# The next tile's rows turned ahead of the last second products, in two PSUM banks of their own, and the experts' bounds told ahead of the tiles' slots

## The chip, the core and the metric

The kernel runs on one core of a Trainium2 chip. A core has a matrix engine (TensorE, PE in the profile; its weight loads are PEld), a vector engine (VectorE, DVE), an activation engine (ScalarE, ACT), a general engine (GpSimd, POOL) and one that issues transfers (SyncE, SP). Each has an instruction queue of its own, and they wait for each other by semaphores. A row marked PEq, DVEq, ACTq, POOLq or SPq shows what an engine's sequencer does itself: register operations, branches, semaphore waits, the issue of transfers. SBUF is the working memory of 128 partitions; PSUM has eight banks of 512 words a partition and takes the products.

The metric is the device time of the whole program in microseconds (us); lower is better.

## The reference

Three stages in a row. A linear attention with a delta rule runs over 768 steps for 4 x 8 heads of 48; its output, 3072 tokens of 384, goes through a dense layer pair (2048 wide, SiLU); then each token is either passed on as it is or gets the output of one of 8 experts (1024 wide, ReLU), weighted by its gate. The change is in the last stage:

```python
def _moe2_ref(x, w_skip, w_gate, w1, w2):
    skip_score = x @ w_skip
    do_compute = skip_score > 0
    out = x.copy()
    ...
    xc = x[do_compute]
    logits = xc @ w_gate
    e_idx = np.argmax(logits, axis=1)
    ...
    for e in range(E):
        mask = e_idx == e
        ...
        h = np.maximum(xc[mask] @ w1[e], 0.0)
        y[mask] = gate_w[mask, None] * (h @ w2[e])
    out[do_compute] = xc + y
```

## The kernel before

Attention and the dense layers are interleaved over chunks of 128 tokens until about 660 us of the profiled execution. They write each token's row (384 values and 8 logits) to a table in memory, x_table, and the token's number to id_table, at a slot in the range of its expert. Then come the experts, in tiles of G2 = 256 tokens. How many tiles each expert has is known only at run time; here it is one each, eight tiles in all.

**The plan (VectorE, lines 1552 to 1567).** One-partition instructions compute from the slots used how many tiles each expert has. They give two rows: `ends` (from which tile to which an expert runs, line 1559), which every engine reads into registers as the bounds of its loops, and `starts` (at which slot each tile begins, lines 1561 to 1567), which only POOL reads, to load a tile's ids (`load_ids_of`, line 761). One semaphore, plan_ready, tells of both; all engines wait for it. Behind the plan VectorE makes xt_lo of tile 0 (line 1570).

**Number format.** A 32-bit operand is split in two, a high and a low part (hi, lo), and each product is made of three: hi by hi, lo by hi, hi by lo (`three` for the first products; lines 1125 to 1127 for the second). ScalarE makes the high part, and VectorE the low one as the difference. For the token rows these are xt_hi and xt_lo, for the hidden layer h_hi and h_lo, for the weights w_hi and w_lo.

**A tile on each engine** (`one`, in a loop over the tiles of an expert, within a loop over pairs of experts; the last two experts stand behind that loop):
- TensorE runs n from 0 to 9. For n < 8 it makes a group of nine first products (w1, 128 of the 1024 columns) in the bank up_ps[n % 2], for n >= 2 a group of six second products (w2) of d = n - 2 into both down_ps. Group n of the first products waits for h_lo of group n - 2, since it takes that group's bank. At n = 8 and n = 9 it first turns half of the next tile's rows (`transposes`: three transposes for each half, by a product with the identity, line 1096) into up_ps[0] and up_ps[1], which no first product needs any more, and then makes the second products of d = 6 and d = 7.
- ScalarE makes h_hi from each group (line 1254), the high parts of the next expert's weights in between (line 1137, w_hi), at n = 2 a copy of the gathered rows (xg), and at the end both xt_hi of the next tile (`xt_parts`). A tile begins with a small operation that brings a table load with it where the pair loop begins (line 1249: three of the eight tiles).
- VectorE makes h_lo (line 1584), the low parts of the next expert's weights (line 1537), the gate, then both xt_lo of the next tile, and last y of this tile in two instructions (line 1602), once all second products are done (edown_done). After that its sequencer goes through the loop's end and reads the next expert's bounds (lines 513, 514) before the next h_lo.
- POOL gathers by indirect DMA the rows of the next tile (line 739), loads the ids of the one after (line 735), and scatters y to the output (line 794). `hold` is a wait followed by a one-element operation (line 684), so that what is behind it in the queue starts late enough. Ahead of the loops it loads the ids of tiles 0 and 1 and gathers the rows of tile 0 (lines 760 to 768); the turned rows of tile 0 are made another way and don't need that gather, but ScalarE's copy in tile 0 does, and POOL gathers tile 1 only when that copy is done.
- SP loads the weights of the expert after next, piece by piece, each as VectorE has split the piece before it in the same buffer (line 650).

In each engine the order of the work is the order of the code, with waits written by hand.

## Time and profile before

| | us |
|---|---|
| median of 3 timed runs | 834.72 (834.37 to 834.73) |
| the profiled execution | 832.83 |
| its span, first to last instruction | 831.2 |
| TensorE busy | 785.8 (95%) |
| VectorE busy | 568.4 (68%) |
| ScalarE busy | 369.3 (44%) |
| POOL busy | 112.3 (14%) |

Tile 0 of the experts begins at 670.08 us, the last tile's products end at about 818.7, and the last rows of the output are stored by 831.2. In the rows further down, a time in front is the start from the beginning of the span, the second number the duration; `[0.21 <-DVE xt_lo L1576]` says that the engine sat idle for 0.21 us before and what released it. A row with x3 merges three instructions, and its duration runs from the first's start to the last's end. Neighbouring instructions of one engine overlap in the records, so a start minus the start before is the pace. L and a number is a line of the kernel before; kv_t holds y, the gates and the scattered rows in this stage, kq_t the gathered rows, bp and dg the weights as loaded, u_sb the plan's rows.

### The profile page before, as it was taken

To read this page: it belongs to the slowest core of one execution; us is meant where nothing else is said; L and a number is where in the kernel's file an instruction comes from. 1 tells how busy PE (TensorE), PEld (TensorE's weight loads), DVE (VectorE), ACT (ScalarE), POOL (GpSimd) and SP (SyncE) were. 2 spreads that over 40 slices of the span, in tenths; PEclk is the share of its full clock that TensorE was granted. 3 is DMA by queue.
4 is the path that set the end of the run, shared out by engine and by line. 5 is a ranking of instruction groups with operands and counts; after the bars stand their busy time and mean duration, and the time that the engine had idled before them with its cause. 6 is when DMAs were issued, how large, how long until landed. Compare 5 with 4: busy or idle time off the path is not lost.

```text
span 831.2 us, 29093 instructions
## 1 busy us (share of the span) xinstructions
PE 785.8 (95%) x12081; PEld 714.4 (86%) x12082; DVE 568.4 (68%) x1504; ACT 369.3 (44%) x1042; POOL 112.3 (14%) x281
## 2 busy tenths in 40 slices
PE   5977999999999999999999999999999989999993
PEld 3545888899989998899999899999999989999993
DVE  6978798868687776778768677655323666767751
ACT  3723433535335343453424444343543565666641
POOL 1000000001020000101002010100104054344441
PEclk9987999999999999999999999999999999999997
DMA  8753121122201213122220211211123646655510
GB/s 270 231 163 124 34 67 53 60 91 66 86 34 66 69 63 100 39 65 72 68 89 24 67 61 48 65 41 47 40 78 122 196 141 196 192 191 185 188 32 15
DMA packets 46649, 79.75 MB, mean 96 GB/s; under 512 B 5680, under 2 KB 35082, under 8 KB 46144
## 3 DMA queue, kind: packets, MB, share of 16 engines
q1 hardware_dynamic: 43104, 73.07, 27.3%
q0 software_dynamic: 3424, 4.93, 1.9%
q8 instruction: 92, 1.51, 0.8%
q14 instruction: 29, 0.24, 0.1%
HBM read 67.05 MB, written 13.19 MB: 97 GB/s over the span
## 4 chain that ended last, share of the span: by engine, by line
issue 79%; POOL 9%; DMA 6%; POOLq 2%; PE 2%; DVE 1%; SPq 0%; ACT 0%
DMA id_table<-token,slot 5%; POOL idle L684 3%; POOL kq_t L739 2%; POOL id_table L729 2%; PE psum L984 1%; POOL ids_all L735 1%; POOL out L794 1%; DMA x_sb<-kq 1%; DMA id_table<-x_sb 0%; POOLq L513 0%; POOLq L514 0%; POOLq L761 0%; PE psum L840 0%; POOL token L722 0%; PE psum L985 0%
## 5 line engine op out<-in xcount | busy, mean ns | idle before, releaser
L1018 PE MATMUL psum<-xt_hi,w_hi 128*128 128x256 f32 x768 | 225.9, 294 | 7.1 <-issue 2.7
L1019 PE MATMUL psum<-xt_lo,w_hi 128*128 128x256 f32 x768 | 217.2, 283 | 0.0
L1020 PE MATMUL psum<-xt_hi,w_lo 128*128 128x256 f32 x768 | 217.0, 283 | 0.0
L1194 ACT ACTIVATE h_raw<-psum 128x256 f32<-128x256 f32 x192 | 73.8, 385 | 309.2 <-PE psum L1020 307.5
L1453 DVE TENSOR_TENSOR h_lo<-h_raw,h_hi 128x256 fp32r<-128x256 f32 x192 | 81.3, 424 | 160.7 <-ACT h_hi L1195 149.8
L1018 PEld LDWEIGHTS psum<-xt_hi,w_hi 128*128 128x128 f32 x768 | 144.8, 189 | 16.8 <-issue 10.8
L1020 PEld LDWEIGHTS psum<-xt_hi,w_lo 128*128 128x128 f32 x768 | 146.0, 190 | 0.0
L1019 PEld LDWEIGHTS psum<-xt_lo,w_hi 128*128 128x128 f32 x768 | 145.4, 189 | 0.0
L1042 PE MATMUL psum<-w_hi,h_hi 128*128 128x394 f32 x384 | 138.7, 361 | 3.0 <-DVE h_lo L1453 2.4
L1044 PE MATMUL psum<-w_hi,h_lo 128*128 128x394 f32 x384 | 131.2, 342 | 0.0
L1043 PE MATMUL psum<-w_lo,h_hi 128*128 128x394 f32 x384 | 131.0, 341 | 0.0
L684 POOL TENSOR_TENSOR idle<-half 1x1 f32<-1x1 f32 x125 | 35.3, 296 | 641.6 <-PE psum L916 484.7
L1137 ACT ACTIVATE u_sb<-psum 32x96 f32<-32x96 f32 (+1 forms) x360 | 88.7, 247 | 25.5 <-PE psum L916 20.5
L1042 PEld LDWEIGHTS psum<-w_hi,h_hi 128*128 128x128 f32 x384 | 72.4, 188 | 9.9 <-DVE h_lo L1453 4.2
L1387 DVE SCALAR_TENSOR_TENSOR bp<-psum,gamma,seen 128x256 f32<-128x256 f32 x192 | 79.2, 475 | 2.4 <-PE psum L1005 2.3
L1195 ACT ACTIVATE h_hi<-psum 128x256 fp32r<-128x256 f32 x192 | 72.6, 378 | 0.0
L1043 PEld LDWEIGHTS psum<-w_lo,h_hi 128*128 128x128 f32 x384 | 72.4, 189 | 0.0
L1044 PEld LDWEIGHTS psum<-w_hi,h_lo 128*128 128x128 f32 x384 | 72.3, 188 | 0.0
L1408 DVE TENSOR_TENSOR inv<-inv,outer 128x30 f32<-128x30 f32 (+9 forms) x180 | 59.9, 333 | 6.2
L1137 ACT ACTIVATE w_hi<-bp 128x768 fp32r<-128x768 f32 (+1 forms) x62 | 58.5, 944 | 9.5 <-DMA bp<-moe_w_in 9.5
L1537 DVE TENSOR_TENSOR w_lo<-bp,w_hi 128x1024 fp32r<-128x1024 f32 (+1 forms) x48 | 52.4, 1092 | 14.8 <-ACT w_hi L1137 14.8
L1405 DVE TENSOR_TENSOR outer<-low,inv 128x30 f32<-128x30 f32 (+9 forms) x180 | 58.8, 327 | 2.9
(183 smaller groups left out, 1100.5 us busy)
## 6 DMA issues: line engine op xcount, KB each, us to landing
kq_t<-kq SPq DMA_DIRECT2D x24, 512.0 KB, 3.6
bp<-moe_w SPq DMA_DIRECT2D x24, 512.0 KB, 5.7
kv_t<-kv SPq DMA_DIRECT2D x24, 384.0 KB, 3.1
bp<-moe_w SPq DMA_DIRECT2D x24, 384.0 KB, 5.1
kd<-kq SPq DMA_DIRECT2D x20, 256.0 KB
x_table<-x_sb SPq DMA_DIRECT2D x13, 392.0 KB, 2.9
out<-x_sb SPq DMA_DIRECT2D x12, 384.0 KB
bp<-moe_w_in SPq DMA_DIRECT2D x6, 512.0 KB, 7.1
```

The lines of the kernel that those rows point to most:

```text
L684: return g.tensor_tensor(idle[:, at:at + 1], half[0:1, 0:1], half[0:1, 0:1], ALU.mult)
L1018: m(out, hi, x_hi, start=first, stop=False)
L1019: m(out, hi, x_lo, start=False, stop=False)
L1020: return m(out, lo, x_hi, start=False, stop=last)
L1042: m(down_ps[a][:, 0:WS], h_hi[:, r, rows], w_hi[1][:, w], start=i == 0, stop=False)
L1043: m(down_ps[a][:, 0:WS], h_hi[:, r, rows], w_lo[1][:, w], start=False, stop=False)
L1044: last = m(down_ps[a][:, 0:WS], h_lo[:, r, rows], w_hi[1][:, w], start=False, stop=i == M1 - 1)
L1137: return a_.activation(out, in_, ACT.Copy, scale=scale)
L1194: a_.activation(h_raw[i % 2][:, :], up_ps[i % 2][:, 0:G2], ACT.Silu)
L1195: a_.activation(h_hi[:, i % RING, :], up_ps[i % 2][:, 0:G2], ACT.Silu).then_inc(h_hi_ready, 1)
L1387: d.scalar_tensor_tensor(bp[t % NB][:, h, :], gram_ps(t, h), gamma[quad(t)][:, at:at + 1], seen[:, h // 2, :], ALU.mult, ALU.mult).then_in ...
L1453: d.tensor_tensor(h_lo[:, i % RING, :], h_raw[i % 2][:, :], f32(h_hi[:, i % RING, :]), ALU.subtract).then_inc(h_lo_ready, 1)
```

## The change

Two banks of PSUM that the expert stage didn't use (6 and 7) take the turned rows (turn_ps), in place of up_ps[0] and up_ps[1]. TensorE turns both halves at n = 8, ahead of the wait for h_lo and of the second products of d = 6; nothing stands ahead of those of d = 7 any more but their own wait. ScalarE and VectorE read the turned rows from the new banks, in the same order among their instructions as before.

In the plan, `ends` is told by plan_ready as soon as it is there, VectorE then makes xt_lo of tile 0, and only behind that come the instructions that compute `starts`, which have a semaphore of their own, starts_ready. POOL waits for that one ahead of line 761.

```diff
@@ -182,6 +182,7 @@
         psum = ctx.enter_context(nc.psum_tensor("psum", [P, 8, 512], F32))
         up_ps = [psum[:, g, :] for g in range(2)]
         down_ps = [psum[:, 2 + g, :] for g in range(2)]
+        turn_ps = [psum[:, 6 + g, 0:KD * C] for g in range(2)]
         first_ps = psum[:, 4:6, :].rearrange("p b (k n) -> p (b k) n", n=G2)
 
 
@@ -251,7 +252,7 @@
             sem, ("route_step", "route_in", "token_ready", "id_stored", "table_blank"))
         out_stored, table_stored = sem("out_stored"), sem("table_stored")
 
-        plan_step, plan_ready = sem("plan_step"), sem("plan_ready")
+        plan_step, plan_ready, starts_ready = map(sem, ("plan_step", "plan_ready", "starts_ready"))
         ids_loaded, xg_gathered, xg_copied, ids_copied = map(sem, ("ids_loaded", "xg_gathered", "xg_copied", "ids_copied"))
         ew_half, ew_split = map(sem, ("ew_half", "ew_split"))
         ew_loaded = [sem(f"ew_loaded{x}") for x in range(len(e_stage))]
@@ -761,7 +762,7 @@
                 load_ids(pool.value_load(starts[0:1, bass.ds(t, 1)], min_val=0, max_val=E * N - G2), ids_in, ids_loaded)
 
             load_ids(0, ids_next, first_in)
-            pool.wait_ge(plan_ready, 1)
+            pool.wait_ge(starts_ready, 1)
             load_ids_of(1)
             pool.wait_ge(table_stored, 16 * NP)
             pool.wait_ge(out_stored, 16 * NP)
@@ -1093,7 +1094,7 @@
             def transposes(t, a):
                 pe.wait_ge(xg_gathered, t * 32 + 32)
                 for x in range(KD):
-                    last = tr(up_ps[a][:, C * x:C * x + C], xg_in[a][:, C * x:C * x + C], ident[:, :])
+                    last = tr(turn_ps[a][:, C * x:C * x + C], xg_in[a][:, C * x:C * x + C], ident[:, :])
                 last.then_inc(xgt_ps[a], 1)
 
             def one(e, i, more):
@@ -1112,13 +1113,14 @@
                                 last = three(up_ps[n % 2][:, 0:G2], w_hi[i][:, w], w_lo[i][:, w], xt_hi[0][:, x, :], xt_lo[0][:, x, :],
                                              x == 0, x == KD - 1)
                             last.then_inc(eup_done, 1)
+                        if n == M2:
+                            for a in range(2):
+                                transposes(t + 1, a)
                         if n >= 2:
                             d = n - 2
                             pe.wait_ge(eh_lo_ready, t * M2 + d + 1)
                             if d == 0:
                                 pe.wait_ge(y_ready, t + 1)
-                            if n >= M2:
-                                transposes(t + 1, n - M2)
                             w = slice(W2_AT + DM * d, W2_AT + DM * d + DM)
                             for a in range(2):
                                 rows, r = slice(C * a, C * a + C), d % RING
@@ -1239,7 +1241,7 @@
             def xt_parts(t):
                 for a in range(2):
                     act.wait_ge(xgt_ps[a], t + 1)
-                    cp(xt_hi[0][:, :, C * a:C * a + C], up_ps[a][:, 0:KD * C].rearrange("p (k c) -> p k c", k=KD)).then_inc(xgt_hi[a], 1)
+                    cp(xt_hi[0][:, :, C * a:C * a + C], turn_ps[a].rearrange("p (k c) -> p k c", k=KD)).then_inc(xgt_hi[a], 1)
 
             def one(e, i, more):
                 first, last_t = expert_bounds(act, e)
@@ -1556,7 +1558,12 @@
             then(d.tensor_scalar(tiles_f, tiles_f, 1.0, None, ALU.max))
             then(d.tensor_tensor(part, earlier, tiles_f.unsqueeze(1).to_broadcast([1, E + 1, E]), ALU.mult))
             then(d.tensor_reduce(ends_f, part, AX.X, ALU.add))
-            d.tensor_copy(ends, ends_f)
+            d.tensor_copy(ends, ends_f).then_inc(plan_ready, 1)
+
+            for b in range(2):
+                dve.wait_ge(xgt_hi[b], 1)
+                d.tensor_tensor(xt_lo[0][:, FIRST[b]:FIRST[b + 1], :], first_ps[:, FIRST[b]:FIRST[b + 1], :],
+                                f32(xt_hi[0][:, FIRST[b]:FIRST[b + 1], :]), ALU.subtract).then_inc(xgt_lo[b], 1)
 
             then(d.tensor_scalar(jump, tiles_f[:, 0:E - 1], -float(G2), float(N), ALU.mult, ALU.add))
             then(d.tensor_tensor(past, tile_no[0:1, :].unsqueeze(2).to_broadcast([1, MAXT + 2, E - 1]),
@@ -1564,16 +1571,11 @@
             then(d.tensor_tensor(past, past, jump.unsqueeze(1).to_broadcast([1, MAXT + 2, E - 1]), ALU.mult))
             then(d.tensor_reduce(starts_f, past, AX.X, ALU.add))
             then(d.scalar_tensor_tensor(starts_f, tile_no[0:1, :], float(G2), starts_f, ALU.mult, ALU.add))
-            d.tensor_scalar(starts, starts_f, float(E * N - G2), None, ALU.min).then_inc(plan_ready, 1)
-            for b in range(2):
-                dve.wait_ge(xgt_hi[b], 1)
-                d.tensor_tensor(xt_lo[0][:, FIRST[b]:FIRST[b + 1], :], first_ps[:, FIRST[b]:FIRST[b + 1], :],
-                                f32(xt_hi[0][:, FIRST[b]:FIRST[b + 1], :]), ALU.subtract).then_inc(xgt_lo[b], 1)
-
+            d.tensor_scalar(starts, starts_f, float(E * N - G2), None, ALU.min).then_inc(starts_ready, 1)
             def xt_parts(t):
                 for a in range(2):
                     dve.wait_ge(xgt_hi[a], t + 1)
-                    d.tensor_tensor(xt_lo[0][:, :, C * a:C * a + C], up_ps[a][:, 0:KD * C].rearrange("p (k c) -> p k c", k=KD),
+                    d.tensor_tensor(xt_lo[0][:, :, C * a:C * a + C], turn_ps[a].rearrange("p (k c) -> p k c", k=KD),
                                     f32(xt_hi[0][:, :, C * a:C * a + C]), ALU.subtract).then_inc(xgt_lo[a], 1)
 
             def one(e, i, more):
```

TensorE, the end of a tile in the last expert, before: kq_t0 and kq_t1 are the two halves of the next tile's gathered rows.

```order
L1127 MATMUL psum<-w_hi1,h_lo 128x384
L1117 REGISTER_ALU
L1094 ISA
L1096 MATMUL psum<-ident,kq_t0 128x128 x3
L1125 MATMUL psum<-w_hi1,h_hi 128x384
L1126 MATMUL psum<-w_lo1,h_hi 128x384
L1127 MATMUL psum<-w_hi1,h_lo 128x384
L1125 MATMUL psum<-w_hi1,h_hi 128x384
L1126 MATMUL psum<-w_lo1,h_hi 128x384
L1127 MATMUL psum<-w_hi1,h_lo 128x384
L1117 REGISTER_ALU
L1096 MATMUL psum<-ident,kq_t1 128x128 x3
```

And the same place of the changed kernel, whose lines have moved by one to two:

```order
L1129 MATMUL psum<-w_hi1,h_lo 128x384
L1095 ISA
L1097 MATMUL psum<-ident,kq_t0 128x128 x3
L1097 MATMUL psum<-ident,kq_t1 128x128 x3
L1121 REGISTER_ALU
L1127 MATMUL psum<-w_hi1,h_hi 128x384
L1128 MATMUL psum<-w_lo1,h_hi 128x384
L1129 MATMUL psum<-w_hi1,h_lo 128x384
L1127 MATMUL psum<-w_hi1,h_hi 128x384
L1128 MATMUL psum<-w_lo1,h_hi 128x384
L1129 MATMUL psum<-w_hi1,h_lo 128x384
L1121 REGISTER_ALU
```

The second half's three transposes have moved ahead of the six second products of d = 6; the twelve second products now stand together, and no instruction has gone or come.

VectorE, the end of the plan, before: L1559 writes `ends`, L1567 `starts`, both in u_sb.

```order
L1559 CAST u_sb<-u_sb 1x9
L1561 TENSOR_SCALAR u_sb<-u_sb 1x7
L1562 TENSOR_TENSOR h_raw<-tile_no,u_sb 1x154
L1564 TENSOR_TENSOR h_raw<-h_raw,u_sb 1x154
L1565 TENSOR_REDUCE u_sb<-h_raw 1x22
L1566 SCALAR_TENSOR_TENSOR u_sb<-tile_no,u_sb 1x22
L1567 TENSOR_SCALAR u_sb<-u_sb 1x22
L1570 TENSOR_TENSOR xt_lo<-psum,xt_hi 128x512
L1570 TENSOR_TENSOR xt_lo<-psum,xt_hi 128x256
```

The same place of the changed kernel:

```order
L1561 CAST u_sb<-u_sb 1x9
L1565 TENSOR_TENSOR xt_lo<-psum,xt_hi 128x512
L1565 TENSOR_TENSOR xt_lo<-psum,xt_hi 128x256
L1568 TENSOR_SCALAR u_sb<-u_sb 1x7
L1569 TENSOR_TENSOR h_raw<-tile_no,u_sb 1x154
L1571 TENSOR_TENSOR h_raw<-h_raw,u_sb 1x154
L1572 TENSOR_REDUCE u_sb<-h_raw 1x22
L1573 SCALAR_TENSOR_TENSOR u_sb<-tile_no,u_sb 1x22
L1574 TENSOR_SCALAR u_sb<-u_sb 1x22
```

Both xt_lo, which wait for ScalarE's xt_hi, have moved ahead of the six instructions that make `starts`.

## Rows read from the trace of the kernel before

**Rows 1.** Lines, 640 us to the end, TensorE: busy, mean ns | idle before, releasers.
```profile
L1018 PE MATMUL psum<-xt_hi,w_hi 128*128 128x256 f32 x218 | 62.9, 288 | 5.3 <-issue 2.7 <-DVE xt_lo L1576 1.5 <-DVE h_lo L1584 1.0
```

**Rows 2.** Timeline, TensorE, from tile 2 to tile 3: start us, us, line, [idle before].
```profile
723.77 0.49 PE L1096 MATMUL psum<-ident,kq_t 128*128 128x128 f32 x3
...
725.15 0.49 PE L1096 MATMUL psum<-ident,kq_t 128*128 128x128 f32 x3
...
726.36 0.34 PE L1127 MATMUL psum<-w_hi,h_lo 128*128 128x384 f32 x1
...
726.91 0.36 PE L1018 MATMUL psum<-xt_hi,w_hi 128*128 128x256 f32 x1 [0.21 <-DVE xt_lo L1576]
...
729.15 0.39 PE L1018 MATMUL psum<-xt_hi,w_hi 128*128 128x256 f32 x1
```

**Rows 3.** Timeline of VectorE there; then its queue's register operations: ns, first and last start.
```profile
725.24 0.56 DVE L1576 TENSOR_TENSOR xt_lo<-psum,xt_hi 128x384 fp32r<-128x384 f32 x1
726.20 0.56 DVE L1576 TENSOR_TENSOR xt_lo<-psum,xt_hi 128x384 fp32r<-128x384 f32 x1 [0.41 <-ACT xt_hi L1137]
726.84 1.14 DVE L1602 SCALAR_TENSOR_TENSOR kv_t<-psum,kv_t,kq_t 128x384 f32<-128x384 f32 x2
728.67 0.42 DVE L1584 SCALAR_TENSOR_TENSOR h_lo<-psum,h_hi 128x256 fp32r<-128x256 f32 x1 [0.69 <-ACT h_hi L1254]
...
L1581 DVEq ALU_OP  x1: 40/40/40, 726.9 to 726.9; - x1
...
L1581 DVEq FUSED_REGOPS  x1: 63/63/63, 728.5 to 728.5; - x1
```

**Rows 4.** The same from tile 1 to tile 2, where the pair loop goes round.
```profile
707.93 1.14 DVE L1602 SCALAR_TENSOR_TENSOR kv_t<-psum,kv_t,kq_t 128x384 f32<-128x384 f32 x2
710.42 0.83 DVE L1584 SCALAR_TENSOR_TENSOR h_lo<-psum,h_hi 128x256 fp32r<-128x256 f32 x2 [1.35 <-ACT h_hi L1254]
...
L1581 DVEq FUSED_REGOPS  x1: 63/63/63, 710.0 to 710.0; - x1
```

**Rows 5.** Timeline of VectorE, then of ScalarE, at the hand-over to tile 0.
```profile
666.11 0.16 DVE L1559 CAST u_sb<-u_sb 1x9 int32<-1x9 f32 x1
666.19 0.15 DVE L1561 TENSOR_SCALAR u_sb<-u_sb 1x7 f32<-1x7 f32 x1
...
667.60 0.17 DVE L1567 TENSOR_SCALAR u_sb<-u_sb 1x22 int32<-1x22 f32 x1
667.69 1.00 DVE L1570 TENSOR_TENSOR xt_lo<-psum,xt_hi 128x512 fp32r<-128x512 f32 x2
...
666.51 0.60 ACT L1137 ACTIVATE xt_hi<-psum 128x512 fp32r<-128x512 f32 x1 [5.05 <-PE psum L1086]
667.37 0.38 ACT L1137 ACTIVATE xt_hi<-psum 128x256 fp32r<-128x256 f32 x1 [0.27 <-PE psum L1086]
```

**Rows 6.** POOL's queue at L761, then the timelines of POOL and SP.
```profile
L761 POOLq TENSOR_LOAD <-u_sb x1: 520/520/520, 668.4 to 668.4; - x1
...
670.49 0.36 POOL L684 TENSOR_TENSOR idle<-half 1x1 f32<-1x1 f32 x2
...
672.79 1.01 POOL L739 DMA_INDIRECT kq_t<-x_table,ids_all  x1 [0.30 <-issue]
...
675.93 0.67 POOL L684 TENSOR_TENSOR idle<-half 1x1 f32<-1x1 f32 x1 [2.13 <-DMA kq_t<-x_table,ids_all]
...
680.85 1.00 POOL L739 DMA_INDIRECT kq_t<-x_table,ids_all  x1 [0.31 <-issue]
...
686.56 0.33 POOL L684 TENSOR_TENSOR idle<-half 1x1 f32<-1x1 f32 x2 [3.96 <-DMA kq_t<-x_table,ids_all]
...
675.28 9.61 SPq L650 DMA_DIRECT2D bp<-moe_w  x6
```

**Rows 7.** Timeline of TensorE: the start of tile 0, and its stop near the end.
```profile
670.08 0.36 PE L1018 MATMUL psum<-xt_hi,w_hi 128*128 128x256 f32 x1 [2.75 <-issue]
...
686.54 0.55 PE L1096 MATMUL psum<-ident,kq_t 128*128 128x128 f32 x3 [1.15 <-DMA kq_t<-x_table,ids_all]
```

## The prediction

> **What bounds the kernel now.** I read the page of the profile first: TensorE is busy for 95% of the span, so only its gaps and the work it waits for can move the time. The grouped lines of the stretch after 640 us then show how little it waits in the experts: 5.3 us ahead of the first products of a group, 2.7 of them "issue", 1.5 behind xt_lo and 1.0 behind h_lo [rows 1]. Third, the timeline of TensorE over one change of tile. The first transposes start at 723.77, the second at 725.15, the last second product at 726.36, the next tile's first product at 726.91, and its third group of first products (n = 2) at 729.15 [rows 2]. That last start is the one to watch. At every one of the eight tiles the third group starts 0.06 us after the first h_lo ends; here h_lo starts at 728.67 and takes 0.42, so it ends at 729.09. Two groups lie between 726.91 and 729.15, and both run without a break, so a tile that begins earlier gains only if its first h_lo comes earlier too.
>
> Fourth, VectorE and its queue at the same place [rows 3]. The two y instructions (L1602) start at 726.84, about 0.14 after the last product's modelled end (726.36 + 0.34). The queue's first register operation at the loop's end follows at 726.9, and the last one of the next tile's head at 728.5. h_lo starts at 728.67, 0.17 later. So the chain from tile to tile is: last second product, y, 1.7 us of register work of VectorE's queue (the bounds are read again for every expert), first h_lo, third group. xt_lo, which the change brings forward, stands beside this chain and not on it.
>
> Last, the hand-over to tile 0: VectorE's plan, ScalarE's xt_hi and POOL's queue [rows 4 to 6].
>
> **The turning of the next tile, part by part.** No instruction is added: six transposes, twelve second products, two xt_hi, two xt_lo, two y. On TensorE three transposes and six products take 725.15 - 723.77 = 1.38, three transposes and five products 726.36 - 725.15 = 1.21; so a product is 0.17 and a transpose about 0.12. All six first take 0.7, and the last product, with eleven ahead of it, starts where it did, at 726.36.
>
> The second transposes end about 1.05 earlier, so the second xt_hi does too, and the second xt_lo follows the first (725.24) at once, 0.48 later, and ends near 726.28 instead of 726.76. TensorE can then go on at 726.53 instead of 726.91: 0.38 per change of tile, seven times. I count none of it directly. y waits for the last product, which hasn't moved, so VectorE's queue is ready when it was: 728.5 plus the operation and a dispatch, about 728.60. h_lo can start 0.07 earlier than 728.67, and TensorE waits the rest at the third group. At the two changes where the pair loop goes round, ScalarE loads a table and holds h_lo longer: y 707.93, last register operation 710.0, h_lo 710.42 [rows 4]; the other one reads alike, with 0.48 in place of 0.42 between the last two. ScalarE starts its table load about 0.9 earlier, since it has both xt_hi behind it, and h_lo falls back on VectorE's queue, 0.3 earlier. At the other five changes h_lo now starts 0.1 to 0.27 after the last register operation, of which about 0.13 can't go: 0 to 0.14 each, together 0.4. Sum: 2 x 0.3 + 0.4 = **1.0 us gained**. If that queue were quicker by a tenth per tile it would be 1.7, if ScalarE's table load still held h_lo, 0.4. The last tile gains nothing: its y waits for the same last product.
>
> **The bounds ahead of the slots.** plan_ready is told after L1559 (starts 666.11, 0.16 long) and not after L1567 (667.60): 1.5 us earlier. Then VectorE waits for xt_hi: ScalarE's two copies are 666.51 + 0.60 and 667.37 + 0.38, ended 667.11 and 667.75 [rows 5]. xt_lo runs from 667.13 to 668.17 (1.00 for the two before, and a little between them), 0.5 earlier than 668.69. TensorE, whose queue now reads the bounds while its last products of the hand-over run, can begin near 668.6 and not at 670.08 [rows 7]. It then meets the same wall: VectorE's queue must pass the six plan instructions left, and so is 0.2 to 0.4 earlier with the first h_lo. And all of it is lost at the end of this tile, where TensorE stands for 1.15 us until the rows of tile 1 land, 686.54 [rows 7]. Worth there: 0.
>
> **What is paid.** The six plan instructions (L1561 to L1567, 666.19 to 667.77, 1.58) now stand behind both xt_lo: they start at 668.09 and end at 669.67. POOL waits for them (starts_ready) ahead of L761, which began at 668.4 [rows 6]. It begins at 669.7: **1.3 later**. Behind it in POOL's queue are the load of tile 1's ids, the gather of tile 0's rows (second half issued at 672.79, landed 675.93), the copy by ScalarE, and the gather of tile 1's rows (second half 680.85, landed 686.56); POOL waits only for these landings on the way, so all shift by 1.3. TensorE's stop at 686.54 becomes 687.84. Behind ScalarE's waiting copy are the fourth h_hi and the weight splits of the next expert; they come 1.3 later too, and TensorE may stop for some 0.4 at the sixth group, but it has that to spare before 687.84. So its gap there is about 2.3 us, less than the 2.75 before 670.08 [rows 7], after which the first product takes 0.36 as at every change of tile [rows 2]; I expect no loss of clock.
> Ends for this cost: nothing, if the gather of tile 0 is held by something else after all; above, 1.3 plus what the weight loads add. The first gather landed 2.1 after its second half had been issued (672.79 + 1.01 long, to 675.93), with no other transfer about; the second, among the weight loads, took 4.7 (680.85 + 1.00, to 686.56). SP issues the first of these loads at 675.28 [rows 6], and the moved gather is issued until 675.1. It could take up to 2.6 more, 3.9 in all. I take 1.4, near the quiet row, as the loads start only when most of its bytes have moved.
> The Trainium skill, DMA: Bandwidth & Descriptors, section Queues, rings and completion order, says that each DMA engine takes turns between its queues packet by packet. By that, a gather that meets the loads is slowed from the first shared packet; the two gathers of rows 6 agree (2.1 and 4.7), and it speaks for the upper end.
>
> **Sum**: -1.0 + 1.4 = +0.4 us on the profiled execution (832.83, span 831.2). The median of the timed runs is 834.72, 1.9 above that execution; the step carries over, and gives 835.1.
>
> **The rivals.**
> 1. The early start counts in full (faster). If VectorE's queue could do its register work while y still waits, the first h_lo would follow h_hi. Then five changes give 0.38 each, and the two with a table load about 0.85, as h_hi behind the earlier table load then sets them; 3.6 in all, less 1.3: 832.4. Against it: at the changes of tile the register operation stands 0.06 to 0.1 after y's start, never before. A chance of 0.08.
> The Trainium skill, Advanced Engine Details and Errata, section Sequencer Loop, has engine instructions waiting in a queue while control instructions go on; by that this rival would win. In rows 3 the register operation at 726.9 does follow y at 726.84, which had a semaphore to wait for, so the row speaks against the rule here.
> 2. The gather falls among the weight loads (slower). The place is the gather of tile 0, the price up to 3.9 in place of 1.4, and it decides once the landing is late by more than 2.7: then the sum passes +1.7. For it: the loads at 675.28. Against: its second half would be written by 675.1, and the loads are paced by splits that shift as well. With 3.8 it gives 837.5. A chance of 0.16; a fallen clock behind the longer stop would add to it.
> 3. The later slots cost nothing (the gather is held by the landing of ids). Then only the 1.0 stays: 833.7. Against: POOL's two holds ahead of that gather stand back to back at 670.49, with no wait between them [rows 6]. A chance of 0.08.
> The forecast has 0.68.
>
> **How the numbers follow.** What a measurement of this kernel can tell is about 0.2%, 1.7 us: faster is below 833.05, slower above 836.39. The forecast (834.2 to 836.2 by its bounds) and nearly all of rival 3 are within; rival 1 is faster, rival 2 mostly slower. That makes 0.11 faster, 0.70 the same, 0.19 slower. The range, 833.3 to 837.2, takes in rival 3 and most of rival 2.
>
> **What would show it.** Right: six transposes together at about 0.7 us, last product and y at the same distance behind them as before; the next tile's first product directly behind the last second product; a new wait of about 0.3 to 0.4 for h_lo ahead of each tile's third group; y to first h_lo still 1.75 to 1.85, and about 2.2 with the pair loop; L761 of POOL near 669.7, TensorE's stop for the rows of tile 1 ending near 687.9. Wrong: h_lo less than 1.7 behind y, no wait at the third group, or L761 near 668.4. If that stop ends after 689.3, rival 2 has it.

## The result and the profile after

| | kernel before | changed kernel |
|---|---|---|
| median, timed side by side (20 runs each) | 833.39 us (830.19 to 835.3) | 835.0 us (833.46 to 838.52) |
| ratio, changed to before | | 1.0027, 95% interval 1.0015 to 1.0039 |
| profiled execution (its span) | 832.83 (831.2) | 835.72 (834.1) |
| TensorE busy | 785.8 | 786.3 |

By the ratio the change costs some 2.3 us. The gain at the changes of tile came out as worked; the loss at tile 0 is more than twice what I had put down.

**A change of tile.** TensorE and VectorE from tile 2 to tile 3, which answer to [rows 2, 3], and then the register operations of VectorE's queue (ns, first and last start):

```profile
727.36 0.82 PE L1097 MATMUL psum<-ident,kq_t 128*128 128x128 f32 x6
...
729.95 0.33 PE L1129 MATMUL psum<-w_hi,h_lo 128*128 128x384 f32 x1
...
732.66 0.39 PE L1019 MATMUL psum<-xt_hi,w_hi 128*128 128x256 f32 x1 [0.24 <-DVE h_lo L1586]
```

```profile
728.83 1.02 DVE L1578 TENSOR_TENSOR xt_lo<-psum,xt_hi 128x384 fp32r<-128x384 f32 x2
730.42 1.14 DVE L1604 SCALAR_TENSOR_TENSOR kv_t<-psum,kv_t,kq_t 128x384 f32<-128x384 f32 x2 [0.58 <-PE psum L1129]
732.18 0.42 DVE L1586 SCALAR_TENSOR_TENSOR h_lo<-psum,h_hi 128x256 fp32r<-128x256 f32 x1 [0.61 <-ACT h_hi L1256]
...
L1583 DVEq ALU_OP  x1: 40/40/40, 730.5 to 730.5; - x1
...
L1583 DVEq FUSED_REGOPS  x1: 63/63/63, 732.1 to 732.1; - x1
```

The two xt_lo run without a pause, y waits for the last product, the register work starts behind it and ends at 732.1, h_lo follows 1.76 behind y, and TensorE, which is ready earlier, waits 0.24 for it. From third group to third group the eight tiles were 18.92, 18.25, 18.90, 18.28, 18.25 and 18.27 apart before, behind tile 1, and are now 18.60, 18.19, 18.59, 18.16, 18.25 and 18.10.

**Tile 0**, which answers to [rows 5 to 7]. VectorE, POOL's queue and POOL, SP, TensorE:

```profile
665.92 0.16 DVE L1561 CAST u_sb<-u_sb 1x9 int32<-1x9 f32 x1
666.96 1.07 DVE L1565 TENSOR_TENSOR xt_lo<-psum,xt_hi 128x512 fp32r<-128x512 f32 x2 [0.88 <-ACT xt_hi L1139]
...
669.36 0.17 DVE L1574 TENSOR_SCALAR u_sb<-u_sb 1x22 int32<-1x22 f32 x1
...
672.18 1.22 DVE L1539 TENSOR_TENSOR w_lo<-bp,w_hi 128x1024 fp32r<-128x1024 f32 x1
```

```profile
L762 POOLq TENSOR_LOAD <-u_sb x1: 520/520/520, 669.6 to 669.6; - x1
...
672.38 1.97 POOL L740 DMA_INDIRECT kq_t<-x_table,ids_all  x1 [0.41 <-issue]
674.66 1.01 POOL L740 DMA_INDIRECT kq_t<-x_table,ids_all  x1 [0.30 <-issue]
678.65 0.18 POOL L685 TENSOR_TENSOR idle<-half 1x1 f32<-1x1 f32 x1 [2.99 <-DMA kq_t<-x_table,ids_all]
...
683.56 1.74 POOL L740 DMA_INDIRECT kq_t<-x_table,ids_all  x1 [0.30 <-issue]
...
688.98 0.33 POOL L685 TENSOR_TENSOR idle<-half 1x1 f32<-1x1 f32 x2 [2.72 <-DMA kq_t<-x_table,ids_all]
...
673.60 12.88 SPq L651 DMA_DIRECT2D bp<-moe_w  x6
```

```profile
668.41 0.36 PE L1019 MATMUL psum<-xt_hi,w_hi 128*128 128x256 f32 x1 [1.25 <-DVE xt_lo L1565]
...
671.91 0.39 PE L1019 MATMUL psum<-xt_hi,w_hi 128*128 128x256 f32 x1 [1.13 <-DVE h_lo L1586]
...
680.33 0.39 PE L1019 MATMUL psum<-xt_hi,w_hi 128*128 128x256 f32 x1 [1.78 <-DVE h_lo L1586]
...
688.96 1.03 PE L1097 MATMUL psum<-ident,kq_t 128*128 128x128 f32 x6 [1.98 <-DMA kq_t<-x_table,ids_all]
...
690.10 0.52 PE L1128 MATMUL psum<-w_lo,h_hi 128*128 128x384 f32 x1
690.42 0.52 PE L1129 MATMUL psum<-w_hi,h_lo 128*128 128x384 f32 x1
```

Read from the top: the bounds are told earlier, tile 0 starts 1.67 earlier than in [rows 7] (0.18 of it is chance: this execution came to the hand-over that much sooner), and the slots are made behind xt_lo; POOL reads them at 669.6. But SP's first weight load has come forward too, from 675.28 to 673.60, before the gather is written. The gather's first half now takes 1.97 in place of 1.07, and its rows land 2.7 later than in [rows 6]. Of the early start little is left at once: TensorE waits 1.13 for h_lo ahead of tile 0's third group, as foreseen. It then stops twice more, 1.78 for h_lo at the sixth group and 1.98 for the rows of tile 1, and behind the last stop its second products stand 0.32 apart and not 0.17. The stretches of that place show why (us, busy time of each engine, granted clock of TensorE, share of DMA, GB/s):

```profile
688.00:690.00 2.00, 1.04 (x7) 1.05 (x8) 0.31 (x3) 0.46 (x1) 0.63 (x4) 0.89 0.87 234
690.00:692.00 2.00, 2.00 (x7) 2.00 (x7) 1.04 (x2) 0.71 (x3) 0.58 (x1) 0.50 0.53 177
692.00:694.00 2.00, 2.00 (x12) 2.00 (x12) 0.36 (x1) 0.00 (x0) 0.00 (x0) 0.76 0.02 1
```

A granted clock of 0.50 is the lower of the two levels, 1.2 GHz. Before the fall TensorE had stood still for 1.98. In the profile shown of the kernel before, the same place stands at 1.00. From the six transposes to y it is 4.68 here and 3.06 at the change of tile above: 1.6 for the clock.

### The profile page after: what moved, and what is told of

It reads as the page before. It is cut to its first block, busy times and chain, and to the rows that moved or that the text cites. A ratio compares the mean times of both kernels' runs of the same rounds, so it can differ in the third digit from the quotient of the medians.

```text
span 834.1 us, 29085 instructions
## 1 busy us (share of the span) xinstructions
PE 786.3 (94%) x12081; PEld 716.4 (86%) x12082; DVE 567.7 (68%) x1504; ACT 368.5 (44%) x1042; POOL 114.3 (14%) x281
## 4 chain that ended last, share of the span: by engine, by line
PE 65%; issue 14%; DVE 8%; POOL 6%; DMA 2%; POOLq 2%; ACT 2%; SPq 0%; ACTq 0%; DVEq 0%
PE psum L1043 9%; PE psum L1019 8%; PE psum L1045 7%; PE psum L1044 7%; PE psum L1021 7%; PE psum L1020 7%; DVE bp L1389 3%; PE psum L917 3%; PE psum L875 2%; POOL idle L685 2%; POOL kq_t L740 2%; PE psum L931 2%; DMA bp<-moe_w_out_t 2%; PE psum L895 2%; PE psum L841 2%
```

## The experiments

Each was timed in five rounds beside the kernel before, except where it says otherwise. Executions differ in when the hand-over to the experts comes (660.11 to 668.05 in these profiles, with nothing of the change ahead of it), so tile 0 is compared from one product on, called the hand-over here: the first of the twelve of L1086 (up to L1089 in the other kernels), the last that TensorE makes ahead of tile 0. The columns from "first gather issued" to "third group of tile 1" are us behind it:

| kernel | hand-over at | first gather issued | its rows land | rows of tile 1 land | third group of tile 1 | clock at 0.50 in tile 0 | ratio |
|---|---|---|---|---|---|---|---|
| before | 664.48 | 6.93 | 11.45 | 22.1 | 27.50 | nowhere | 1 |
| before, again | 666.57 | 7.15 | 11.60 | 23.2 | 28.61 | at the start of tile 0 | |
| turning alone | 667.47 | 7.10 | 11.56 | 22.9 | 28.24 | at the start | 0.9982 |
| turning alone, again | 662.90 | 7.16 | 12.46 | 23.6 | 30.47 | behind the stop | 0.9983 |
| turning, gather delayed a little | 660.11 | 7.21 | 11.63 | 20.8 | 27.32 | at the start | 0.9982 |
| turning, gather delayed | 662.55 | 8.14 | 15.04 | 24.4 | 30.04 | behind a stop | 0.9995 |
| turning, y at the head | 663.20 | 7.18 | 12.48 | 23.6 | 30.11 | behind the stop | 0.9952 |
| y at the head alone | 664.32 | 7.30 | 11.70 | 23.3 | 29.08 | at the start | 1.0034 |
| **changed** | 664.30 | 8.08 | 14.35 | 24.7 | 31.57 | behind a stop | 1.0027 |
| plan alone | 665.42 | 8.16 | 14.83 | 25.1 | 30.50 | behind a stop | 1.0027 |
| changed, loads held | 664.16 | 8.14 | 13.45 | 24.8 | 31.59 | behind a stop | 1.0022 |
| changed, slots first | 668.05 | 8.03 | 15.07 | 26.0 | 31.39 | behind a stop | 1.0044 |
| slots first, loads held | 667.23 | 8.40 | 13.78 | 25.3 | 32.23 | behind a stop | 1.0046 |
| y at the head, slots first, loads held | 666.93 | 8.40 | 13.81 | 25.3 | 31.85 | behind a stop | 1.0015 |

**1. The turning alone, and the plan alone.** Each is the kernel before with one half of the diff.

> The kernel before with only the two banks and the early transposes; plan and semaphores as before. Theory A (the change of tile is held by VectorE's register work between y and the first h_lo; the loss of the whole change sits in tile 0 and comes from the plan): third group to third group shrinks by 0.3 us at the two changes with a table load and by 0 to 0.15 at the others, about 1.0 in all; tile 0 starts near 670.1 and its stop for the rows of tile 1 ends near 686.5, as before; the clock stays at 1.00. Time about 1.0 us (0.1%) below before, 'same' by the bound. Theory B (the early transposes themselves cost, for instance the clock falls because all products stand together): slower than before, with a granted clock under 1.00 in tile 0. Rival of the forecast (the early start counts in full): 3 us below.

> The kernel before with only the plan part: ends told first, xt_lo, then starts with a semaphore of its own; transposes in the old place. Theory A: all of the loss is here. The whole change's trace had the third group of tile 1 3.9 us later than before; I expect 3.5 to 4 here too, SP's first weight load near 673.6 in place of 675.3, the gather of tile 0's rows landing near 678.6, TensorE's stop ending near 689, and a granted clock of 0.5 behind it; time about 3.5 us (0.4%) above before, so about 1 above the whole change. Theory B (the loss comes with the turning): no more than 1.4 above.

Measured: turning 832.42, ratio 0.9982 (0.9966 to 0.9998), and run once more 0.9983 (0.9961 to 1.0004); plan 836.19, ratio 1.0027 (1.0009 to 1.0044). The gain is the turning's, and the plan loses 2.3 alone, less than the 3.5 expected. Beside the turning it loses 1.0027 against 0.9982, 3.7 us. The turning's tile 0 was not that of the kernel before, as I had expected: its clock fell in both profiles (table).

> The turning alone once more, on the same chip as turn_y_head. The first profile of it had a lowered clock in the first products of tile 0 (0.86 granted from 668 to 680). Expected: ratio 0.998 again, 1.0 to 1.6 below the kernel before; the periods from third group to third group 18.6 and 18.2 again, and, if the clock was chance, the tile 0 of the kernel before (27.5 from first own product to the third group of tile 1).

**2. Weight loads held until the gather has landed.**

```diff
             sp.wait_ge(plan_ready, 1)
+            sp.wait_ge(xg_gathered, 32)
```

> The whole change, and SP waits until the rows of tile 0 have landed before it issues the first weight load of the loop. Theory A (the earlier start of tile 0 brings the weight loads 1.7 us forward, into the gather that the plan has made 1.3 later): the gather of tile 0 lands about 1.3 to 1.5 later than before (677.3), POOL's gather instruction takes 1.0 and not 1.97, the gather of tile 1 lands near 688, TensorE's stops together are under 3 us and the clock stays at 1.00; about 1.5 to 2.5 us below the whole change. Theory C (the gather is late only because starts are late, the loads don't matter): the landing stays near 678.6 and the time is that of the whole change, or later because the loads are.

```profile
672.30 1.94 POOL L741 DMA_INDIRECT kq_t<-x_table,ids_all  x1 [0.47 <-issue]
674.55 1.01 POOL L741 DMA_INDIRECT kq_t<-x_table,ids_all  x1 [0.30 <-issue]
677.61 0.18 POOL L686 TENSOR_TENSOR idle<-half 1x1 f32<-1x1 f32 x1 [2.05 <-DMA kq_t<-x_table,ids_all]
```

This is POOL with the loads held (first load at 678.88). The landing behind the second half takes 2.05 and not 2.99: the loads cost the gather 0.9. But the first half is as long as in the changed kernel, and the loads now fall into the gather of tile 1, which lands when it did. Ratio 1.0022 (1.0005 to 1.004): nothing won of the 1.5 to 2.5 expected.

**3. The slots first again, with the bounds still told early**, once with the loads free and once held.

```diff
             d.tensor_copy(ends, ends_f).then_inc(plan_ready, 1)
-            for b in range(2):          # both xt_lo
-                ...
             then(d.tensor_scalar(jump, tiles_f[:, 0:E - 1], -float(G2), float(N), ALU.mult, ALU.add))
             ...
             d.tensor_scalar(starts, starts_f, float(E * N - G2), None, ALU.min).then_inc(starts_ready, 1)
+            for b in range(2):          # both xt_lo
+                ...
```

> The whole change with xt_lo of tile 0 behind starts again, ends still told first: starts ready at 667.8 as before, all engines read their bounds 1.5 us earlier. Theory A: POOL's load of starts is back at 668.4; TensorE can begin tile 0 near 668.9, so the weight loads still come forward, by about 1.2; they then meet a gather that is 1.3 earlier than in the whole change, and collide less: its landing near 676 to 677, TensorE's stop ending near 686.5 to 687.5, clock 1.00. Time 2.5 to 3.5 us below the whole change, about 0.5 to 1 below before. Theory C (only starts matter): the same with the landing at 675.9 exactly as before.

> The changed kernel with two differences: the six instructions that make the slots run ahead of xt_lo again (the bounds still told before them), and SP waits for the gathered rows of tile 0 (xg_gathered at 32) ahead of its first weight load. It is the fourth corner of a square: slots early or late, weight loads among the gather or behind it. Theory A, the early weight loads cost: the gather lands about 2.1 us behind the issue of its second half, not 5.7 as in slots_first; TensorE's stop for the rows of tile 1 ends near 22.5 to 23 behind its first own product of the hand-over (before 22.1, changed 24.7, slots_first 26.0), the clock stays up, and the time is 1.5 to 2.5 below the changed kernel: near 832.5 to 833.5, ratio about 0.9995 to the kernel before. Theory B, the loads are only moved into the gather of tile 1, which pays it back: the first gather lands quickly, the second takes 5 or more, the stop ends near 24.5 as in loads_held, and the time is near 835.5, ratio 1.002.

Measured: 837.1, ratio 1.0044 (1.002 to 1.0069), and 835.93, ratio 1.0046 (1.0023 to 1.0069). Both theories of the first failed, and theory A of the second; its theory B (1.002) was nearer. Early bounds with the slots first lose at least as much as the whole edit. But the gather is as late as before (issued at 8.03 and 8.40), so no run here has early bounds and a gather on time. POOL of the kernel with the loads held, and its transfers from 671.7 to 673.3 (queues: packets, MB, share):

```profile
671.95 0.59 POOL L737 DMA_DIRECT2D ids_all<-id_table  x1
673.29 0.56 POOL L737 DMA_DIRECT2D ids_all<-id_table  x1 [0.75 <-issue]
...
674.90 0.18 POOL L686 TENSOR_TENSOR idle<-half 1x1 f32<-1x1 f32 x1 [0.85 <-DMA ids_all<-id_table]
675.63 1.90 POOL L741 DMA_INDIRECT kq_t<-x_table,ids_all  x1 [0.55 <-issue]
...
q8 instruction: 1, 0.02, 4.0%
```

In [rows 6] the two holds ahead of the gather begin at 670.49, 1.92 behind the issue of tile 0's ids, and end without a wait for them. Here the second hold waits, until 2.95 behind that issue; with the loads free it was 3.27, with y at the head 3.12. In those 1.6 us one packet of 16 KB is read by the queue that brings instructions, while the ids come; in the kernel before no such packet stands in the same stretch, it comes 1.1 to 1.7 later. The other profiles divide the same way. In all six with early bounds that packet starts 4.9 to 5.5 behind the hand-over, and the ids land 2.9 to 3.2 behind their issue; in all eight with the old bounds it starts 6.6 to 7.3 behind it, and they land in 2.0 to 2.3. That the packet holds back the ids is likely, but only argued: no run moved it alone. In the changed kernel the ids were late too (landed 7.27 behind the hand-over), but the hold for them began at 7.49, so there they cost nothing. These three profiles came late to the hand-over (666.9 to 668.1), as did one of the turning alone (667.47); that is ahead of anything that differs.

**4. A late gather with the old bounds.** The turning alone, and idle operations of POOL ahead of the load of tile 1's ids (seven, then thirteen).

```diff
             pool.wait_ge(plan_ready, 1)
+            for _ in range(13):
+                hold(plan_ready, 1)
             load_ids_of(1)
```

> The turning alone (plan as before), and seven one-element operations of POOL (about 0.18 us each, 1.26 together) ahead of the load of tile 1's ids: the gather of tile 0 is issued as late as in the changed kernel, but the bounds are told at the old time, so TensorE and SP's weight loads start when they did. Theory A, the late gather costs by itself, and more than its own shift, because it then starts inside VectorE's w_lo: the first gather instruction takes 1.8 to 2.0 us instead of 1.07, both halves are issued by 11.3 behind the first own product of the hand-over (9.5 in turn_only), the stop for the rows of tile 1 ends 2 us later than in turn_only and turn_again, near 25 behind that product, and the time is 1.5 to 2.3 above turn_only: ratio to the kernel before about 1.0005. Theory B, only the early bounds cost: the first gather stays near 1.1 long or its length doesn't reach the stop, and the time is within 0.7 of turn_only, ratio 0.998 to 0.999.

> As late_gather, with thirteen one-element operations of POOL in place of seven. Seven ran in 1.05 us beside 0.75 of the queue's own work, and the gather started at 7.21 behind the first own product of the hand-over (turn_again 7.16), so nothing had been tested; thirteen should take 1.95 and start it 1.1 to 1.2 later, at 8.2 to 8.4, as in the changed kernel (8.08), with the bounds still told at the old time. Theory A, the late slots cost by themselves: the gather meets VectorE's w_lo and takes more than 1.07, it is the later by 1.2 to 2 at its landing, TensorE stops at the sixth group for h_lo by 0.3 or more, the third group of tile 1 is 29.5 or more behind that product, and the time is 1.2 to 2 above the turning alone: ratio 1.000 to 1.001. Theory B, it is the early bounds (TensorE and the weight loads 1.3 to 1.7 earlier) that cost: the ratio stays 0.998 to 0.999.

Seven told nothing: they ran beside 0.75 of POOL's own queue work, and the gather wasn't late (7.21, ratio 0.9982). Thirteen moved it to 8.14 and gave 833.04, ratio 0.9995 (0.997 to 1.0019), some 1 above the turning alone, with intervals that overlap, so that this price is likely and not shown. TensorE stopped 2.22 for h_lo at the sixth group, as in the changed kernel. POOL and VectorE there:

```profile
670.69 1.08 POOL L740 DMA_INDIRECT kq_t<-x_table,ids_all  x1 [0.16 <-issue]
672.07 2.00 POOL L740 DMA_INDIRECT kq_t<-x_table,ids_all  x1 [0.30 <-issue]
...
671.97 1.22 DVE L1541 TENSOR_TENSOR w_lo<-bp,w_hi 128x1024 fp32r<-128x1024 f32 x1 [0.52 <-ACT w_hi L1141]
```

This time the second half is the long one, and the first is not. It is the half that starts inside a w_lo: 672.07 lies in 671.97 to 673.19. In the changed kernel 672.38 lies in the w_lo of 672.18, and 683.56 in one of 683.48. The fourteen profiles hold 252 such halves. The 164 that start while no w_lo runs, or in its last 0.03, take 1.00 to 1.08, also where one follows 0.05 to 0.15 later; 21 of them start inside an h_lo, which reads only one operand from SBUF, and take 1.00 to 1.03. Of the other 88 three start within 0.05 of a w_lo's start and take 1.01; with 0.2 to 0.27 of w_lo left they take 1.08 to 1.15, with 0.35 left 1.22, with 0.45 left 1.32, with 0.87 left 1.74, with 0.93 to 1.12 left 1.83 to 2.00. So the gather waits for the rest of w_lo, less some 0.13. That rule comes from counting in the traces, not from an edit that took w_lo away.

**5. Is VectorE's queue the wall?** y of a tile moves in VectorE's program from the end of the body to the head of the next one, behind the register reads.

```diff
                 with dve.Fori(first, last_t) as t:
+                    y_of(t)
                     for x in range(M2):
                         ...
-                    dve.wait_ge(edown_done, t * M2 + M2)
-                    for a in range(2):
-                        last = d.scalar_tensor_tensor(y_sb[a], ...)
-                    last.then_inc(y_ready, 1)
+            y_of(dve.value_load(ends[0:1, E:E + 1], min_val=1, max_val=MAXT))
```

Of the edit this leaves out: a y that nobody uses now stands ahead of tile 0's first h_lo, so the other engines' waits for y and for the second products count one more.

> The turning alone (plan as before), and in VectorE's program y of a tile has moved from the end of the loop body to the head of the next one, behind the sequencer's register reads and branches; y of the last tile stands behind the loops. Theory A, the 1.7 us of register work between y and the next h_lo is a wall that holds back each tile: now that work is done while VectorE waits for the last product, h_lo starts 1.2 to 1.3 behind y's start, the wait ahead of the third group goes, and each of the seven changes of tile gains 0.2 to 0.4 more (up to 0.85 with a table load): 2.0 to 2.6 below turn_only (832.42), 830 to 830.4, ratio about 0.9955. Theory B, something else sets h_lo (h_hi of ScalarE, or y itself, 1.14 long): then the third group still waits as long behind a different releaser, and the time is within 0.7 of turn_only.

> The kernel before with only y moved to the head of the next tile's body in VectorE's program; turning and plan as before. turn_y_head was at 0.9952 and the turning alone at 0.998. Theory A, the two need each other: without the turning TensorE can't start the next tile earlier (xt_lo holds it), so the wall's removal frees nothing but the two changes with a table load, 0.3 each, and the 0.06 to 0.1 behind each h_lo: 0.5 to 1.2 below before, ratio 0.9987 to 0.9995. Theory B, they add up: the head alone is worth what was measured of it on top of the turning, 2.5 to 3, ratio 0.997.

> turn_y_head with the bounds told early as well, the slots made ahead of xt_lo, and SP's first weight load held until the rows of tile 0 have landed. If the early start of tile 0 is worth something once the gather isn't disturbed, this is at or up to 1 us below turn_y_head (near 829.5); if all of it is lost at the stop for the rows of tile 1, as I predicted and as loads_held suggests, it is equal to turn_y_head or up to 2 us above it, by the later loads falling into the gather of tile 1.

With the turning: 828.29, ratio 0.9952 (0.9933 to 0.997), faster than both kernels. Without it: 835.47, ratio 1.0034 (1.0017 to 1.0051). VectorE with the turning, then without, both from tile 2 to tile 3:

```profile
725.82 1.02 DVE L1579 TENSOR_TENSOR xt_lo<-psum,xt_hi 128x384 fp32r<-128x384 f32 x2
727.69 1.14 DVE L1585 SCALAR_TENSOR_TENSOR kv_t<-psum,kv_t,kq_t 128x384 f32<-128x384 f32 x2 [0.85 <-PE psum L1129]
728.80 0.42 DVE L1595 SCALAR_TENSOR_TENSOR h_lo<-psum,h_hi 128x256 fp32r<-128x256 f32 x1
...
L1591 DVEq ALU_OP  x1: 40/40/40, 726.0 to 726.0; - x1
...
L1591 DVEq FUSED_REGOPS  x1: 63/63/63, 727.6 to 727.6; - x1
```

```profile
727.77 0.56 DVE L1577 TENSOR_TENSOR xt_lo<-psum,xt_hi 128x384 fp32r<-128x384 f32 x1 [0.41 <-ACT xt_hi L1137]
729.54 1.15 DVE L1583 SCALAR_TENSOR_TENSOR kv_t<-psum,kv_t,kq_t 128x384 f32<-128x384 f32 x2 [1.21 <-issue]
730.60 0.41 DVE L1593 SCALAR_TENSOR_TENSOR h_lo<-psum,h_hi 128x256 fp32r<-128x256 f32 x1
...
L1589 DVEq ALU_OP  x1: 40/40/40, 727.9 to 727.9; - x1
...
L1589 DVEq FUSED_REGOPS  x1: 63/63/63, 729.4 to 729.4; - x1
```

With the turning y still waits for TensorE, so the register work (726.0 to 727.6) lies beside the last products, and h_lo starts 1.11 behind y where it was 1.76 to 1.83. The traces bear out the time: the six periods from third group to third group are together 2.35 shorter than those of the turning alone. Without the turning the second xt_lo waits for ScalarE until 727.77, the register work begins only behind its start, 727.9, and y waits for "issue", 1.21, and not for a product: the register work and then y's 1.15 now stand between xt_lo and h_lo. The six periods are 1.63 longer than before. Neither theory had a slower kernel. Each edit needs the other: -1.4 and +2.8 us apart, -4.0 together. With early bounds and held loads added the gain is gone again: 1.0015 (0.9995 to 1.0035), 5.2 above the same kernel without them, where 2 was the most that I expected. Its six periods are as short, so that loss sits in tile 0 too.

**6. The kernel before, a second profile** (one execution, 836.03 us).

> The kernel before once more, for a second profile of it. In the first one the clock stayed at 1.00 through tile 0 and the rows of tile 1 landed 22.1 behind the first own product of the hand-over. All nine other profiles had one stretch at 0.50 there, those with the old plan too. If the first was the exception, this one has a stretch at 0.50 near 686 to 692 and the third group of tile 1 is 28.5 to 30.5 behind the first own product; if the old order of the end of a tile keeps the clock up, it is 27.5 again at 1.00.

The clock fell here too, but ahead of the stop: first products 0.41 long from 673.17, and

```profile
672.00:676.00 4.00, 3.81 (x20) 3.84 (x21) 0.43 (x1) 1.47 (x4) 2.90 (x5) 0.59 0.14 32
```

TensorE reached the stop for the rows of tile 1 later and waited 0.87 there; the third group of tile 1 stands at 28.61, as expected, but the fall isn't where I had expected it. The first profile, with no fall in tile 0, was the exception among fourteen.

## Why the prediction came out as it did

The time given, 835.1, was met (835.0), but that is luck: it stood on the median first shown (834.72), the kernel before measured 833.39 beside the changed one, and this 1.3 too much hid a cost that was 1.9 too low. By the ratio the change costs 2.3 and I had 0.4: within 0.2% was the forecast, and it is 0.27%.

- **The turning, gained 1.0: right.** The changes of tile gave 0.32 + 0.06 + 0.31 + 0.12 + 0 + 0.17 = 0.98 on the six periods above. The last product stands 2.59 behind the first transpose, as before; y to h_lo is still 1.76, the new waits are 0.16 to 0.3 (0.3 to 0.4 expected), and 0.65 where ScalarE loads a table. By time the turning alone is worth 1.4 to 1.5.
- **The wall: right, and shown.** y waits and the register operation follows 0.1 behind it at every change; with that work moved ahead of y, 2.6 us more came out (0.9952 against 0.9983). The wall is the wait and not the queue as such: with y at the head the register operations start at 726.0, while the second xt_lo, ahead of them in the program, still stands behind the first. So VectorE's sequencer runs on past an instruction that waits for its engine, but not past one whose semaphore hasn't come. Rival 1 expected 3.6 in all with no such edit; 4.0 is there, but only behind it.
- **L761 at 669.7: right** (669.6). **"All shift by 1.3": wrong.** The first half of the gather started only 1.0 later, but took 0.9 more, since it now started inside a w_lo, the landing behind the second half another 0.9, and the rows came 2.7 later.
- **"Worth there: 0" for tile 0's early start: wrong, it was below nothing.** I had followed the early start to TensorE alone. I took the weight loads at 675.28 as fixed; they are released by VectorE's splits, which start with the tile, and came to 673.60, worth 0.9 of the landing. Two profiles with the old bounds paid as much there (2.9 behind the second half, turning again and y at the head with it), so part of this may be chance. The w_lo that the gather met came forward with them.
- **"Some 0.4 at the sixth group": mis-sized, 1.78.** ScalarE's copy waited for the landing, h_hi and h_lo stood behind it, and TensorE, early, got there sooner.
- **"I expect no loss of clock": wrong, 1.6 us against the profile shown.** I reasoned from the length of one gap, and from the one profile without a fall. With the old bounds the fall came at the start of tile 0 in four of eight profiles, where TensorE had room ahead of its stop; with the new ones, whose gap there is 1.25 to 1.5 and not 2.77, in none of six, and in all six at a stop or behind it: in four the one for the rows of tile 1, behind which nothing can take the loss up, in two (plan alone; slots first) the one at the sixth group. Three of the eight with the old bounds fell behind a stop as well. That is a count, and no experiment forced the clock; what it adds to the cost against a usual execution of the kernel before isn't known.
- **Rival 2** had the slower side and 0.16. Its price (3.8) is near what was paid, and its sign for the splits ("they shift as well") was the wrong way round. By its own signs it is at the edge: the landing was 2.7 later, its condition, but TensorE's stop ended at 688.96 and not after 689.3. Of the 4.1 that tile 0 lost between the two profiles (31.57 against 27.50), the table lets some 1.5 be chance: 30.50 to 32.23 for the early bounds, 27.32 to 30.47 for the late ones, means 31.5 and 28.9.

How the cost divides is settled only in part. The late gather alone is some 1.0 (0.9995 against 0.9983, intervals overlap) of the 3.7 that the plan costs beside the turning, so the larger part is probably the early bounds, or the two together. How much of that is the loads, the w_lo that is met and the clock stays open; holding the loads gave back nothing.

w_lo has two SBUF inputs and the gather reads its ids from SBUF; the 1.97, 2.00 and 1.74 of halves that began inside a w_lo, and the 1.07 of those that began 0.15 ahead of one, agree. The same section infers that a tensor_tensor doesn't stall a DMA that GpSimd issues; for this gather the counts above say that it does. I hadn't weighed it.

## What to carry to other kernels

An instruction that is moved earlier brings everything that it releases with it: list the transfers and the copies on shared ports, not only the engine that was waiting. Where a stop further on swallows a gain, the earlier start isn't worth nothing; it can be worth less. Take a register or branch stretch of a queue as an instruction of its own, and place it where its engine waits anyway: ahead of the wait, not behind it. And where one profile has no lowered clock, take a second before resting a term on that.

## What the runs showed of the hardware that I had not expected

- An indirect gather of POOL takes 1.00 to 1.08 us a half, and up to 2.00 where it starts inside a w_lo of VectorE, but not inside an h_lo (1.00 to 1.03).
- The queue that brings instructions reads a packet of 16 KB 0.5 to 1.7 us behind the start of tile 0. It comes earlier with the bounds, and the ids loaded then land in 2.9 to 3.2 and not 2.0 to 2.3.
- VectorE's register operations pass an instruction that is only queued behind another (726.0 in the kernel with y at the head), not one that waits for a semaphore.
- Thirteen of fourteen profiles had a granted clock of 0.50 once in tile 0. Behind the last stop the fall costs 1.6. At the start of tile 0 (with the old bounds) it puts that tile's third group at 8.79 to 9.35 and not 7.85 to 7.88, but the stop for the rows takes up what it can: tile 1's third group then stands at 27.32 to 29.08, against 27.50 without a fall.
